# Attention and two MoE layers on one core: the inverse sums travel through DRAM, halves are added on VectorE, and the attention stage gets a new order

## The chip, the cores and the metric

One program on one NeuronCore of a Trainium2 chip. The metric is the device time of the whole program in microseconds, as the median of several runs. The kernel before takes 1170.56 us (three runs, 1170.41 to 1171.14).

## The reference

Thirty-two heads (batch 4 by 8 heads) of 576 positions by 64 channels, in float32:

```
q_rot, k_rot = rotate(q), rotate(k)
scores = q_rot @ k_rot.T / sqrt(64)
attn   = exp(scores - max); attn /= sum(attn) + 1e-9
x      = (attn @ v) laid out as 2304 tokens x 512
h = x @ w_in;  g = s * relu(h)**2 + b;  x = g @ w_out      # 512 -> 2048 -> 512
h = x @ w_in2; g = h * sigmoid(1.702 h); out = g @ w_out2  # 512 -> 2048 -> 512
```

## The kernel before

Every float32 operand of a large product is split in a high and a low part of type fp32r, and a product is two or three matmuls of parts. The program has an attention stage (0 to about 355 us) and a layer stage (from there to the end). The layer stage is a dense row of matmuls at L725 and L753 and is hardly touched by the change, except at its start: its first weights are split in `split_w` (Whi on ScalarE, Wlo on another engine), `first_w` does that for the first two blocks of weights inside the attention stage, and the other blocks are loaded by SyncE after its attention work.

The attention stage works on 16 pairs of heads (`p`), h = 0 and 1 within a pair. 576 rows are four full tiles of 128 (j = 0 to 3) and a tail of 64; the tails of both heads share one tile (T). The jobs of a pair are:

- load (SyncE, q, k and v from DRAM into raw and vraw), rot (GpSimd, rotation into rot), prep (TensorE, transposes of rot), qk and klo (ScalarE and VectorE: high and low part of the transposed q and k), qcopy and kcopy (SyncE: copies within SBUF that lay the parts side by side);
- S (TensorE, scores of one tile), max (VectorE, negated row maximum), exp (ScalarE, exponential with the row's sum), all three for eight tiles and for T;
- X (TensorE, transposes of the exponentials), hi (ScalarE) and lo (VectorE), the two parts of the result;
- V and vlo (GpSimd, parts of v), PV (TensorE, 20 matmuls of one head). The high part of v stands in one half of the 128 output rows and the low part in the other, so the result of a head is the sum of two halves of 64 rows;
- evac (ScalarE, all 128 rows of PV's PSUM tile to O), rest (SyncE, a DMA that brings one half of O to the other half's partitions), add (GpSimd, the sum of the halves, osum);
- inv (VectorE, reciprocal of the nine columns of sums), widen (ScalarE, each inverse repeated over 64 columns), B (TensorE, five transposes, which make rows of the inverses in PSUM), finish (VectorE, osum times these rows, into xT).

Each engine runs its jobs in an order written by hand: PE_ORDER, ACT_ORDER, DVE_ORDER, POOL_ORDER and SP_ORDER are lists of one step, and a token such as `S00@1` means the job S of head 0, tile 0, for the pair one ahead of the step. `program` (L82) runs the list for each step. Engines meet only through semaphores.

All results of TensorE pass through four PSUM tiles (slots) of two banks. SLOTS names the slot of each TensorE job, in the order of PE_ORDER. A job waits in `freed` (L172) until the last reader of the job that had its slot before is through: exp for S, lo for X, klo for prep, evac for PV, finish for B. So the order of the jobs and their slots decide who waits for whom.

Of the kernel before, what the change touches and what calls it, by code (L numbers as in the profile page):

```python
# [5 lines left out]
F32 = mybir.dt.float32  # L6
# [4 lines left out]
P = 128  # L11
# [19 lines left out]
def fused_kernel(nc, q, k, v, w1_in, w1_out, w_s, w_b, w2_in, w2_out,  # L31
# [17 lines left out]

    TILES = 2 * NM + 1  # L50
# [38 lines left out]
    JOBS = ("S", "ST", "X", "XT", "PV", "prep", "B")  # L89
# [13 lines left out]
    with outer:  # L103
# [62 lines left out]
        rest_in = [sem(f"rest_in{i}") for i in range(2)]  # L166
        added = sem("added")
        scale_set = sem("scale_set")
        eps_done = sem("eps_done")
        inv_step = sem("inv_step")  # L170
        inv_done = sem("inv_done")
        b_done = sem("b_done")  # L172
        x_done = sem("x_done")

        def freed(eng, job):

            if job is None:
# [59 lines left out]
        def first_w(eng, s, hi):  # L237

            if s == NPAIR - 1:
                eng.wait_ge(prep_t, 2 * NPAIR)  # L240
                eng.wait_ge(v_lo, 2 * NPAIR)
                for i in range(AHEAD):
                    split_w(eng, i, hi)

        with ExitStack() as ctx:
# [33 lines left out]
            O = [sb(f"O{i}", [P, S]) for i in range(2)]  # L279
            rest = sb("rest", [P, S])  # L280
            osum = sb("osum", [P, S])
            inv = sb("inv", [P, NM, 2, D])
            inv_c = sb("inv_c", [P, 2 * NM + 1])
# [32 lines left out]
            def attention_sync(sp):  # L316
# [58 lines left out]
                program(SP_ORDER, {"load": load, "loadv": load_next_v, "qcopy": q_copies, "kcopy": k_copy, "rest": load_rest}, after)  # L375

            def attention_gpsimd(pool):
# [11 lines left out]
                made = {}  # L389

                def rotate_one(p, h, _):
                    g = 2 * p + h
                    if g > 0:
                        pool.wait_ge(qk_in[h], (96 if h == 0 else 32) * (p + 1))
                        rotate(pool, g, byc, bys, rot_step, rotated, g - 1)
                        made[rotated] = g

                def hi_V(p, h, _):
# [3 lines left out]
                    made[v_hi] = 2 * p + h + 1  # L402

                def lo_V(p, h, _):
                    pool.wait_ge(v_hi, 2 * p + h + 1)
                    pool.tensor_tensor(V[h][:, :, 1 - h, :], vraw[:, h, :, :], V[h][:, :, h, :].bitcast(F32), ALU.subtract).then_inc(v_lo, 1)
                    made[v_lo] = 2 * p + h + 1

                def add(p, h, _):

                    pool.wait_ge(evac_done, 2 * p + h + 1)
                    pool.wait_ge(rest_in[h], 16 * (p + 1))
                    need(pool, x_done, p)
                    r = rows_of(h)
                    if h == 0:
                        pool.tensor_tensor(osum[r, :], O[0][r, :], rest[r, :], ALU.add).then_inc(added, 1)
                    else:

                        for signal in made:
                            pool.wait_ge(signal, made[signal])  # L420
                        pool.tensor_tensor(osum[r, 0:MAIN], O[1][r, TAIL:S], rest[r, TAIL:S], ALU.add)
                        pool.tensor_tensor(osum[r, MAIN:S], O[1][r, 0:TAIL], rest[r, 0:TAIL], ALU.add).then_inc(added, 1)
                        pool.wait_ge(added, 2 * p + 2)
                    made[added] = 2 * p + h + 1
# [3 lines left out]
                def after(s):  # L428
                    if 0 <= s - 9 < KT:
                        first_x(pool, s - 1, False)  # L430
                        made[x_lo] = s - 8

                program(POOL_ORDER, {"rot": rotate_one, "V": hi_V, "vlo": lo_V, "add": add}, after)

            def attention_tensor(pe):
# [79 lines left out]
                def B_job(p, _, __):  # L515

                    pe.wait_ge(inv_done, p + 1)
                    freed(pe, before[("B", p, 0, 0)])
                    ps, r = banks("B"), ROW[0]
                    pe.transpose(ps[:, r + MAIN:r + MAIN + P], inv_c[:, 2 * NM:2 * NM + 1].broadcast_to([P, P]), id_sb[:])  # L520
                    for t in range(NM):
                        both = inv[:, t, :, :].rearrange("p h d -> p (h d)")
                        mm = pe.transpose(ps[:, r + t * P:r + (t + 1) * P], both, id_sb[:])  # L523
                    mm.then_inc(b_done, 1)

# [10 lines left out]

                program(PE_ORDER, {"S": S_job, "ST": ST_job, "X": X_job, "XT": XT_job, "PV": PV, "prep": prep_job, "B": B_job})

            def attention_scalar(act):
# [13 lines left out]
                def expT(p, _, __):  # L553
                    c = 2 * NM
# [46 lines left out]
                program(ACT_ORDER, {"exp": exp, "expT": expT, "hi": hi, "hiT": hiT, "evac": evac, "qk": qk, "widen": widen},  # L601
                        after)

            def attention_vector(dve):
                def rowmax(p, h, j):
                    c = NM * h + j
                    dve.wait_ge(s_done, 2 * NM * p + c + 1)
# [4 lines left out]
                def rowmaxT(p, _, __):  # L612
                    c = 2 * NM
# [12 lines left out]
                def invert(p, _, __):  # L626
# [5 lines left out]
                    need(dve, b_done, p)  # L632
                    dve.reciprocal(inv_c[:], sums_eps[:]).then_inc(inv_step, 1)

                def finish(p, _, __):
                    if p < NPAIR - 1:
                        finish_pair(p)

                def finish_pair(p):
                    b, t = p // KT * S, p % KT  # L640
                    ps, r = banks("B"), ROW[0]
                    dve.wait_ge(b_done, p + 1)
                    dve.wait_ge(added, 2 * p + 2)
                    dve.tensor_tensor(xT[:, t, b:b + MAIN], ps[:, r:r + MAIN], osum[:, 0:MAIN], ALU.mult)
                    for h in range(2):
                        at = r + MAIN + h * TAIL
                        last = dve.tensor_tensor(xT[rows_of(h), t, b + MAIN:b + S], ps[rows_of(h), at:at + TAIL],
                                                 osum[rows_of(h), MAIN:S], ALU.mult)
                    last.then_inc(x_done, 1)

                def qk_low(p, h, _):
# [14 lines left out]
                program(DVE_ORDER, {"max": rowmax, "maxT": rowmaxT, "lo": lo, "loT": loT, "inv": invert, "finish": finish,  # L666
                                    "klo": qk_low}, lambda s: first_w(dve, s - 1, False))
                return finish_pair

        with ExitStack() as ctx:  # L670
# [125 lines left out]
            with nc.Block() as block:  # L796
# [51 lines left out]
                def _(dve):  # L848
                    finish_pair = attention_vector(dve)
                    dve.wait_ge(sb_in, 32)  # L850
                    dve.wait_ge(pv_done, 2 * NPAIR)
                    for n in range(STEPS):
# [12 lines left out]
                        if n == 2:  # L865
                            finish_pair(NPAIR - 1)
# [46 lines left out]
```

## Time and profile before

| | us |
|---|---|
| median of three runs | 1170.56 |
| the profiled execution | 1169.46 |
| its span, first to last instruction | 1167.6 |
| TensorE matmuls busy | 1111.2 (95%) |
| TensorE weight loads busy | 1049.7 (90%) |
| VectorE busy | 547.8 (47%) |
| ScalarE busy | 512.0 (44%) |
| GpSimd busy | 237.8 (20%) |
| mean granted TensorE clock | 0.995 of full speed |

The shares over the whole span mix two stages. In the attention stage VectorE, ScalarE and GpSimd are each busy about three quarters of the time and TensorE about 93%. In the layer stage TensorE is busy 100% and the others about a third, GpSimd not at all. The profile is read in this order: busy time by stretch, TensorE's waits in the attention stage, the chain of work that ended last over one step of it, then the durations of the operations that the change touches, and SyncE's DMA issues.

### The profile page before, as it was taken

The page shows a single profiled execution, that of the slowest core. Times are in us where ns is not written, and L with a number is a line of the kernel's source. Part 1 is how long each engine was busy: PE and PEld are TensorE (multiplying, and loading weights), DVE is VectorE, ACT ScalarE, POOL GpSimd, SP SyncE. Part 2 cuts the span into 40 slices and gives each one's busy share as a digit, 9 for nine tenths or more (in the row PEclk, how much of TensorE's full clock was granted, in tenths as well). Part 3 has the DMA queues.
Part 4 walks back from the last instruction along what each step waited for, and adds up shares of the span by engine and source line. Part 5 has one row for each costly group of instructions (what it writes and reads, how often), then busy time and mean ns, then how long its engine had stood idle before and what let it go on. Part 6 is the DMA issues. An engine that isn't in the chain of part 4 may idle for free.

```text
span 1167.6 us, 17056 instructions
## 1 busy us (share of the span) xinstructions
PE 1111.2 (95%) x6608; PEld 1049.7 (90%) x6608; DVE 547.8 (47%) x890; ACT 512.0 (44%) x1015; POOL 237.8 (20%) x254
## 2 busy tenths in 40 slices
PE   3899999999988999999999999999999999999997
PEld 3788888888888999999999999999999999999996
DVE  3677777777765643333333335543232323233222
ACT  2777777777764533232332335532222223222222
POOL 5776867777431000000000000000000000000000
PEclk9899999999999999999999999999999999999999
DMA  6555655545313310000000003400000000000000
GB/s 136 122 121 112 147 127 121 123 110 125 73 26 118 126 55 1 1 1 1 1 1 1 1 1 109 127 19 1 28 1 28 1 1 28 1 28 1 28 1 28
DMA packets 96417, 60.60 MB, mean 52 GB/s; under 512 B 62672, under 2 KB 84048, under 8 KB 96336
## 3 DMA queue, kind: packets, MB, share of 16 engines
q1 hardware_dynamic: 95584, 59.27, 20.4%
q8 instruction: 53, 0.87, 0.3%
q10 hardware_dynamic: 752, 0.23, 0.1%
q14 instruction: 28, 0.23, 0.1%
HBM read 31.16 MB, written 4.72 MB: 31 GB/s over the span
## 4 chain that ended last, share of the span: by engine, by line
PE 90%; ACT 3%; issue 2%; DVE 2%; DMA 1%; POOL 1%; SPq 0%; ACTq 0%; POOLq 0%
PE psum L753 34%; PE psum L725 34%; PE psum L511 8%; PE psum L446 4%; PE psum L477 4%; PE psum L474 2%; PE psum L461 1%; PE psum L533 1%; ACT ET L557 1%; ACT QK L580 1%; DVE QK L653 1%; PE psum L493 1%; PE psum L523 1%; ACT E L550 0%; PE psum L531 0%
## 5 line engine op out<-in xcount | busy, mean ns | idle before, releaser
L725 PE MATMUL psum<-xhi,Whi 128*128 128x384 f32 x768 | 258.4, 336 | 3.6 <-DVE Wlo L218 3.6
L725 PE MATMUL psum<-xhi,Wlo 128*128 128x384 f32 x768 | 258.5, 337 | 0.0
L725 PE MATMUL psum<-xlo,Whi 128*128 128x384 f32 x768 | 258.0, 336 | 0.0
L725 PEld LDWEIGHTS psum<-xhi,Whi 128*128 128x128 f32 x768 | 144.5, 188 | 8.1 <-DVE Wlo L218 4.0
L725 PEld LDWEIGHTS psum<-xlo,Whi 128*128 128x128 f32 x768 | 144.4, 188 | 4.0
L725 PEld LDWEIGHTS psum<-xhi,Wlo 128*128 128x128 f32 x768 | 144.5, 188 | 0.0
L861 DVE SCALAR_TENSOR_TENSOR glo<-act,sb_sb,ghi 128x384 fp32r<-128x384 f32 x96 | 60.1, 626 | 148.1 <-ACT ghi L841 148.1
L753 PE MATMUL psum<-ghi,Whi 128*128 128x384 f32 x384 | 128.9, 336 | 0.0
L753 PE MATMUL psum<-glo,Whi 128*128 128x384 f32 x384 | 128.8, 335 | 0.0
L753 PE MATMUL psum<-ghi,Wlo 128*128 128x384 f32 x384 | 128.6, 335 | 0.0
L841 ACT ACTIVATE ghi<-act,sb_sb 128x384 fp32r<-128x384 f32 x96 | 59.2, 617 | 158.2 <-PE psum L753 154.3
L864 DVE TENSOR_TENSOR glo<-act,ghi 128x384 fp32r<-128x384 f32 x96 | 53.7, 559 | 152.3 <-ACT ghi L843 152.3
L843 ACT CAST ghi<-act 128x384 fp32r<-128x384 f32 x96 | 49.3, 513 | 157.3 <-PE psum L753 157.3
L753 PE MATMUL psum<-Wlo,ghi 128*128 128x512 f32 x288 | 114.0, 396 | 0.0
L753 PE MATMUL psum<-Whi,glo 128*128 128x512 f32 x288 | 113.8, 395 | 0.0
L550 ACT ACTIVATE E<-psum,negmax 128x576 f32<-128x576 f32 x128 | 95.0, 743 | 42.7 <-DVE negmax L610 41.0
L620 DVE TENSOR_TENSOR Xlo<-psum,Xhi 128x576 fp32r<-128x576 f32 x128 | 93.4, 751 | 40.7 <-ACT Xhi L564 40.7
L753 PE MATMUL psum<-Whi,ghi 128*128 128x512 f32 x288 | 112.0, 389 | 0.0
L858 DVE TENSOR_TENSOR act<-psum,act 128x384 f32<-128x384 f32 x96 | 53.5, 558 | 123.9 <-ACT act L837 123.9
L610 DVE TENSOR_REDUCE negmax<-psum 128x1 f32<-128x576 f32 x128 | 95.3, 748 | 32.8 <-PE psum L446 31.1
L837 ACT ACTIVATE act<-psum 128x384 f32<-128x384 f32 x96 | 47.2, 492 | 129.4 <-PE psum L725 129.4
L446 PE MATMUL psum<-QK,Q 128*128 128x320 f32 (+1 forms) x512 | 96.0, 317 | 5.3 <-ACT E L550 3.4
(90 smaller groups left out, 1853.6 us busy)
## 6 DMA issues: line engine op xcount, KB each, us to landing
Q<-QK SPq DMA_DIRECT2D x64, 144.0 KB, 2.5
QK<-QK SPq DMA_DIRECT2D x32, 288.0 KB, 3.3
wraw<-in_moe_w_in_dram SPq DMA_DIRECT2D x32, 256.0 KB, 2.8
wraw<-in_moe_w_out_dram SPq DMA_DIRECT2D x32, 256.0 KB, 3.1
rest<-O SPq DMA_DIRECT2D x32, 144.0 KB, 2.3
raw<-in_q_dram SPq DMA_DIRECT2D x32, 128.0 KB, 2.8
raw<-in_k_dram SPq DMA_DIRECT2D x32, 128.0 KB, 2.5
vraw<-in_v_dram SPq DMA_DIRECT2D x32, 128.0 KB, 2.4
```

Of the source, the lines that this page charges most:

```text
L446: mm = pe.matmul(ps[:, a:b], Q[h][p % 2][:, at:at + P], QK[h][p % 2][:, part, c:c + b - a], start=part == 0, stop=part == 1)
L511: mm = pe.matmul(ps[:, a:b], V[h][:, j, :, :].rearrange("p a d -> p (a d)"), x, start=j == 0 and n == 0, stop=j == NM and n == 1)
L550: act.activation(E[p % 2][:, j, h, :], row(banks("S", h, j), h), ACT.Exp, bias=negmax[p % 2][:, c:c + 1], accum_out=sums[p % 2][:, c:c + 1 ...
L610: dve.tensor_reduce(negmax[p % 2][:, c:c + 1], row(banks("S", h, j), h), AX_X, ALU.max, negate=True).then_inc(max_done, 1)
L620: dve.tensor_tensor(Xlo[h][:, j, :], row(banks("X", h, j), h), Xhi[h][:, j, :].bitcast(F32), ALU.subtract).then_inc(et_lo, 1)
L725: mm = pe.matmul(hps(n), w[i][:, kt * P:(kt + 1) * P], x[C % 2][:, kt, :], start=kt == 0 and j == 0, stop=kt == KT - 1 and j == 2)
L753: mm = pe.matmul(dst, lhsT, rhs, start=i == 0 and j == 0, stop=i == NF - 1 and j == 2)
L841: act.activation(ghi[n % 2][:], a[:], ACT.Identity, bias=sb_sb[:, 1:2]).then_inc(g_hi, 1)
L843: act.copy(ghi[n % 2][:], a[:]).then_inc(g_hi, 1)
L858: dve.tensor_tensor(a[:], hps(n), a[:], ALU.mult).then_inc(g_done, 1)
L861: dve.scalar_tensor_tensor(glo[n % 2][:], a[:], sb_sb[:, 1:2], ghi[n % 2][:].bitcast(F32), ALU.add, ALU.subtract).then_inc(g_lo, 1)
L864: dve.tensor_tensor(glo[n % 2][:], a[:], ghi[n % 2][:].bitcast(F32), ALU.subtract).then_inc(g_lo, 1)
```

## The change

- B and widen are gone. The inverses of a pair (`inv`, 128 by 9) are written to DRAM by one DMA (`put_inv`) as nine rows of 128, element by element, and read back by three DMAs (`get_inv`) as one row of 576 per head, repeated over the 64 partitions of that head, into `inv_row`. The columns of sums are renumbered (COL) so that the tails' column stands between the heads.
- rest and add are gone. evac copies only the 64 rows of its own head; `total` (the token sum) on VectorE adds the other half straight from PSUM. A slot of PV is free after sum, no longer after evac.
- finish is one multiplication of 128 by 576 on GpSimd.
- All five orders, the slots and the order of the banks are new. `first_w` is spread over two steps, and its low parts move from VectorE to GpSimd. finish of the last pair no longer stands in VectorE's layer loop.

```diff
-    PE_ORDER = order("S12@0 prep0@2 S13@0 X00@0 X01@0 S00@1 S01@1 ST@1 prep1@2 S02@1 S03@1 X02@0 X03@0 S10@1 PV1@-1 "
-                     "X10@0 X11@0 XT@0 X12@0 X13@0 B@-1 S11@1 PV0@0")
-    ACT_ORDER = order("hi13@-1 exp11@0 widen@-1 evac0@-1 qk0@2 exp12@0 hi00@0 exp13@0 hi01@0 exp00@1 exp01@1 qk1@2 "
-                      "expT@1 exp02@1 exp03@1 hi02@0 hi03@0 exp10@1 evac1@-1 hi10@0 hi11@0 hiT@0 hi12@0")
-    DVE_ORDER = order("max01@0 lo01@-1 maxT@0 max02@0 klo1@1 max03@0 max10@0 lo02@-1 lo03@-1 lo10@-1 lo11@-1 loT@-1 "
-                      "lo12@-1 inv@-1 max11@0 lo13@-1 finish@-2 max12@0 klo0@2 max13@0 lo00@0 max00@1")
-    POOL_ORDER = order("V0@0 add0@-1 vlo0@0 rot0@3 rot1@3 V1@0 add1@-1 vlo1@0")
-    SP_ORDER = order("loadv1@-3 loadv0@-2 load1@0 qcopy1@-1 kcopy0@-1 rest1@-4 kcopy1@-1 load0@1 rest0@-3 qcopy0@0")
-    SLOTS = [2, 3, 1, 0, 3, 2, 0, 1, 2, 3, 0, 1, 2, 3, 0, 1, 3, 2, 0, 1, 3, 2, 0]
-    SLOT_ORDER = (2, 1, 0, 3)
+    PE_ORDER = order("X01@-1 S01@0 S02@0 X02@-1 S03@0 X03@-1 prep1@1 ST@0 S10@0 S11@0 S12@0 S13@0 PV1@-2 prep0@2 "
+                     "X10@-1 XT@-1 X11@-1 X12@-1 X13@-1 PV0@-1 S00@1 X00@0")
+    ACT_ORDER = order("qk0@2 hi10@-1 hiT@-1 hi11@-1 hi12@-1 hi13@-1 evac0@-1 hi00@0 hi01@0 exp00@1 exp01@1 hi02@0 "
+                      "exp02@1 hi03@0 qk1@2 exp03@1 expT@1 exp10@1 exp11@1 exp12@1 exp13@1 evac1@-1")
+    DVE_ORDER = order("max10@0 max11@0 max12@0 max13@0 sum1@-2 klo0@2 lo10@-1 loT@-1 lo11@-1 lo12@-1 inv@-1 lo13@-1 "
+                      "sum0@-1 max00@1 lo00@0 max01@1 lo01@0 max02@1 lo02@0 max03@1 lo03@0 klo1@2 maxT@1")
+    POOL_ORDER = order("vlo1@-1 V0@0 finish@-2 rot0@3 vlo0@0 V1@0 rot1@3")
+    SP_ORDER = order("loadv1@-2 qcopy0@0 kcopy0@0 qcopy1@0 load1@1 kcopy1@0 put@-3 loadv0@-1 get@-3 load0@2")
+    SLOTS = [0, 2, 3, 1, 0, 2, 1, 3, 0, 2, 1, 3, 0, 1, 3, 2, 0, 1, 3, 2, 1, 3]
+    SLOT_ORDER = (1, 3, 2, 0)
...
         def first_w(eng, s, hi):
 
-            if s == NPAIR - 1:
-                eng.wait_ge(prep_t, 2 * NPAIR)
-                eng.wait_ge(v_lo, 2 * NPAIR)
-                for i in range(AHEAD):
-                    split_w(eng, i, hi)
+            i = s - (NPAIR - 2)
+            if 0 <= i < AHEAD:
+                if hi:
+                    eng.wait_ge(rotated, 2 * NPAIR - 1)
+                    eng.wait_ge(prep_t, 2 * NPAIR)
+                if i == 1:
+                    eng.wait_ge(v_lo, 2 * NPAIR)
+                split_w(eng, i, hi)
...
+                def put_inv(p, _, __):
+                    sp.wait_ge(inv_done, p + 1)
+                    need(sp, inv_in[p % 2], 48 * (p // 2))
+                    sp.dma_start(inv_dram[p % 2].rearrange("t p -> p t"), inv[p % 2][:], allow_slow_non_contiguous=True).then_inc(inv_out[p % 2], 16)
+
+                def get_inv(p, _, __):
+                    sp.wait_ge(inv_out[p % 2], 16 * (p // 2 + 1))
+                    need(sp, x_done, p)
+                    flat = inv_dram[p % 2].rearrange("t p -> (t p)")
+                    for h, at, a, n in ((0, 0, 0, S), (1, MAIN, S, TAIL), (1, 0, S + TAIL, MAIN)):
+                        sp.dma_start(inv_row[rows_of(h), at:at + n],
+                                     flat[a:a + n].rearrange("(o q) -> o q", o=1).to_broadcast([D, n])).then_inc(inv_in[p % 2], 16)
...
+                def finish(p, _, __):
+                    b, t = p // KT * S, p % KT
+                    pool.wait_ge(sum_done, 2 * p + 2)
+                    pool.wait_ge(inv_in[p % 2], 48 * (p // 2 + 1))
+                    pool.tensor_tensor(xT[:, t, b:b + S], osum[p % 2][:], inv_row[:], ALU.mult).then_inc(x_done, 1)
...
+                def total(p, h, _):
+
+                    dve.wait_ge(evac_done, 2 * p + h + 1)
+                    if h == 0:
+                        need(dve, x_done, p - 1)
+                    ps, r = banks("PV", h)[rows_of(1 - h), ROW[h]:ROW[h] + S], rows_of(h)
+                    if h == 0:
+                        last = dve.tensor_tensor(osum[p % 2][r, :], ps, O[r, :], ALU.add)
+                    else:
+                        dve.tensor_tensor(osum[p % 2][r, 0:MAIN], ps[:, TAIL:S], O[r, TAIL:S], ALU.add)
+                        last = dve.tensor_tensor(osum[p % 2][r, MAIN:S], ps[:, 0:TAIL], O[r, 0:TAIL], ALU.add)
+                    last.then_inc(sum_done, 1)
```

## Rows read from the trace of the kernel before

**Rows 1.** Busy time by stretch: start:end, length, each engine's busy us, clock, DMA share, GB/s.
```profile
200.00:300.00 100.00, 93.13 (x705) 85.85 (x704) 76.65 (x124) 76.92 (x162) 76.39 (x79) 1.00 0.51 113
```

**Rows 2.** Waits of TensorE, 100 to 300 us: who waited for whom, total, times, longest.
```profile
PE psum L474 <- DVE QK L653: 6.1, 10, 0.6
PE psum L474 <- ACT ET L557: 4.6, 10, 0.5
```

**Rows 3.** The chain that ended last, in time: start, us, what (B at 209.89).
```profile
209.89 0.28 PE psum L520
...
210.61 0.71 PE psum L446 x4
211.32 2.82 PE psum L511 x20
214.13 0.53 PE psum L446 x4
```

**Rows 4.** Groups of instructions, 100 to 300 us: busy us, mean ns, idle before.
```profile
L610 DVE TENSOR_REDUCE negmax<-psum 128x1 f32<-128x576 f32 x79 | 59.1, 748 | 18.0 <-PE psum L446 16.8
L550 ACT ACTIVATE E<-psum,negmax 128x576 f32<-128x576 f32 x78 | 58.0, 743 | 25.6 <-DVE negmax L610 24.5
L620 DVE TENSOR_TENSOR Xlo<-psum,Xhi 128x576 fp32r<-128x576 f32 x79 | 57.6, 750 | 22.5 <-ACT Xhi L564 22.5
...
L550 ACT ACTIVATION_READ_ACCUMULATOR E<-psum,negmax 128x1 f32 x78 | 15.4, 197 | 0.0
...
L416 POOL TENSOR_TENSOR osum<-O,rest 64x576 f32<-64x576 f32 x10 | 14.1, 1414 | 23.1 <-issue 23.1
...
L574 ACT COPY O<-psum 128x576 f32<-128x576 f32 x20 | 12.8, 640 | 16.7 <-PE psum L511 16.7
```

**Rows 5.** Timelines of VectorE, ScalarE, TensorE near 196 us: start, duration, [idle before <-releaser].
```profile
195.72 0.82 DVE L653 SCALAR_TENSOR_TENSOR QK<-psum,qk_scale,QK 128x576 fp32r<-128x576 f32 x1 [0.56 <-ACT QK L580]
196.46 0.75 DVE L610 TENSOR_REDUCE negmax<-psum 128x1 f32<-128x576 f32 x1
197.12 0.75 DVE L620 TENSOR_TENSOR Xlo<-psum,Xhi 128x576 fp32r<-128x576 f32 x1
...
197.24 0.74 ACT L550 ACTIVATE E<-psum,negmax 128x576 f32<-128x576 f32 x1 [0.30 <-DVE negmax L610]
...
196.60 0.33 PE L474 MATMUL psum<-id_sb,ET 128*128 128x128 f32 x1 [0.61 <-DVE QK L653]
```

**Rows 6.** Timelines of VectorE and GpSimd: the small addition of inv, twice.
```profile
48.66 0.16 DVE L630 TENSOR_TENSOR sums_eps<-sums,eps 128x9 f32<-128x9 f32 x1
...
211.04 0.42 DVE L630 TENSOR_TENSOR sums_eps<-sums,eps 128x9 f32<-128x9 f32 x1
...
210.15 1.29 POOL L421 TENSOR_TENSOR osum<-O,rest 64x512 f32<-64x512 f32 x1 [1.24 <-DMA rest<-O]
```

**Rows 7.** Timeline of SyncE's queue: DMA issues, start and time taken.
```profile
228.56 0.60 SPq L352 DMA_DIRECT2D QK<-QK  x1
...
229.83 1.59 SPq L331 DMA_DIRECT2D raw<-in_q_dram  x2
```

**Rows 8.** DMA issues of the whole run: count, KB each, median us from issue to landing.
```profile
Q<-QK SPq DMA_DIRECT2D x64, 144.0 KB, 2.5
...
raw<-in_k_dram SPq DMA_DIRECT2D x32, 128.0 KB, 2.5
...
raw<-in_k_dram SPq DMA_DIRECT2D x32, 16.0 KB, 2.1
```

**Rows 9.** Timelines: X10 of pairs 0 and 14; load and first matmul of weight block 2.
```profile
44.48 0.30 PE L474 MATMUL psum<-id_sb,ET 128*128 128x128 f32 x1 [1.65 <-DVE Xlo L620]
...
327.52 0.27 PE L474 MATMUL psum<-id_sb,ET 128*128 128x128 f32 x1
...
355.71 0.58 SPq L205 DMA_DIRECT2D wraw<-in_moe_w_in_dram  x1
...
362.87 0.45 PE L725 MATMUL psum<-xhi,Whi 128*128 128x384 f32 x1 [3.64 <-DVE Wlo L218]
```

More of the change, by code:

```diff
@@ L86, in program @@
                 after(s)
[L89 removed]
+    JOBS = ("S", "ST", "X", "XT", "PV", "prep")
     SLOT = {(kind, h, j): slot for (kind, h, j, _), slot in zip([t for t in PE_ORDER if t[0] in JOBS], SLOTS)}
@@ L277, in fused_kernel @@
             sums_eps = sb("sums_eps", [P, 2 * NM + 1])
[L279 to L283, printed above, removed]
+            O = sb("O", [P, S])
+            osum = [sb(f"osum{i}", [P, S]) for i in range(2)]
+            inv = [sb(f"inv{i}", [P, 2 * NM + 1]) for i in range(2)]
+            inv_row = sb("inv_row", [P, S])
+            inv_dram = [nc.dram_tensor(f"inv_dram{i}", [2 * NM + 1, P], F32, kind="Internal").ap() for i in range(2)]
             q_h = q.rearrange("b h s d -> (b h) s d")
@@ L374, in attention_sync @@
                 sp.dma_start(sb_sb[:, 1:2], w_b.rearrange("(a b) -> a b", a=1).to_broadcast([P, 1])).then_inc(sb_in, 16)
-                program(SP_ORDER, {"load": load, "loadv": load_next_v, "qcopy": q_copies, "kcopy": k_copy, "rest": load_rest}, after)
+                program(SP_ORDER, {"load": load, "loadv": load_next_v, "qcopy": q_copies, "kcopy": k_copy, "put": put_inv, "get": get_inv}, after)
             def attention_gpsimd(pool):
@@ L406, in lo_V @@
                     pool.tensor_tensor(V[h][:, :, 1 - h, :], vraw[:, h, :, :], V[h][:, :, h, :].bitcast(F32), ALU.subtract).then_inc(v_lo, 1)
[L407 to L424, printed above, removed]
+                def finish(p, _, __):
[3 more added lines that the diff above has]
+                    pool.tensor_tensor(xT[:, t, b:b + S], osum[p % 2][:], inv_row[:], ALU.mult).then_inc(x_done, 1)
                 pool.wait_ge(tabs_in, 96)
                 def after(s):
[L429 to L433, printed above, removed]
+                    first_x(pool, s - 1, False)
+                    first_w(pool, s - 1, False)
+                program(POOL_ORDER, {"rot": rotate_one, "V": hi_V, "vlo": lo_V, "finish": finish}, after)
             def attention_tensor(pe):
@@ L513, in PV @@
                     mm.then_inc(pv_done, 1)
[L515 to L524, printed above, removed]
                 def prep_job(p, h, _):
@@ L599, in after @@
                     first_w(act, s, True)
-                program(ACT_ORDER, {"exp": exp, "expT": expT, "hi": hi, "hiT": hiT, "evac": evac, "qk": qk, "widen": widen},
+                program(ACT_ORDER, {"exp": exp, "expT": expT, "hi": hi, "hiT": hiT, "evac": evac, "qk": qk},
                         after)
@@ L631, in invert @@
                     dve.wait_ge(eps_done, p + 1)
[L632 to L649, printed above, removed]
+                    need(dve, inv_out[p % 2], 16 * (p // 2))
+                    dve.reciprocal(inv[p % 2][:], sums_eps[:]).then_inc(inv_done, 1)
+                def total(p, h, _):
[9 more added lines that the diff above has]
+                    last.then_inc(sum_done, 1)
                 def qk_low(p, h, _):
@@ L665, in attention_vector @@
                 dve.wait_ge(scale_set, 1)
-                program(DVE_ORDER, {"max": rowmax, "maxT": rowmaxT, "lo": lo, "loT": loT, "inv": invert, "finish": finish,
-                                    "klo": qk_low}, lambda s: first_w(dve, s - 1, False))
-                return finish_pair
+                program(DVE_ORDER, {"max": rowmax, "maxT": rowmaxT, "lo": lo, "loT": loT, "inv": invert, "sum": total,
+                                    "klo": qk_low})
         with ExitStack() as ctx:
```

48 lines of the change are left out of this document (17 added, 31 removed).

## The prediction

> **What bounds the kernel now.** The busy times by stretch come first. In the attention stage TensorE is busy 93 us in 100 and the three others 77 each [rows 1], so no single engine is the bound; the order of the jobs is. The step repeats: between X10 of pair 0 at 44.48 and X10 of pair 14 at 327.52 [rows 9] lie 14 steps, 20.2 us each; the undisturbed ones in the middle take 20.3. TensorE's waits say where its 7% go: once a step it stands 0.6 us for klo and once 0.5 us for expT [rows 2]. The chain of work shows what the rest is: TensorE's own jobs. From the third block of the layers (362.87, rows 9) to the end TensorE never pauses, and no line of that is changed. So the change is worth what it does to 14 steps, to the fill before them and to the turn into the layers.
>
> **What B costs.** B starts at 209.89 and the next job at 210.61 [rows 3], so 0.72 us, and the S behind it takes 0.71 where one behind a PV takes 0.53. TensorE loses 0.9 us of work per pair. That is 14 us if TensorE stayed the bound. It does not, as the walk below shows.
>
> **Work moved.** VectorE gives up finish and takes up sum0 and sum1. All three read 576 columns of PSUM in one to three pieces; lo does that in one piece in 0.75 [rows 4], and for a further small piece I add 0.15 of estimate. So VectorE gains two times 0.75 and loses one time 0.75 and the smaller pieces: some 0.5 us a pair more. ScalarE gives up widen (512 columns, about like evac's 576); evac has half the rows and the same columns, and I keep its 0.64 [rows 4]. GpSimd gives up two adds over 576 columns, 1.41 each, and takes one multiplication of 576 columns, 1.41 by the same row [rows 4]. Each of the three was busy 77% of a step of 20.3, 15.6 us [rows 1]; VectorE comes to 16.1, the others to less. None fills a step, so the order decides again, and I walk through the new one.
>
> **Prices of the walk.** The walk goes job by job through the new lists: a job starts when its engine is free, its data are there and, on TensorE, its slot is. Back to back, VectorE's operations start 0.66 apart (196.46 to 197.12, rows 5) though each lasts 0.75; klo 0.74. A dependent on another engine waits for the end: klo at 195.72 plus 0.82, TensorE starts at 196.60, 0.06 later; max at 196.46 plus 0.75, exp at 197.24, 0.03 later [rows 5]. So max to exp 0.78, lo to TensorE 0.81, klo to TensorE 0.88, evac to sum 0.67, hi to lo the same. exp to TensorE is 0.74 plus the reading of the sum, 0.9 in all [rows 4]. On ScalarE exps start 0.72 apart, hi and evac 0.55, qk 0.64. On TensorE: S 0.53 [rows 3], or 0.63 after a wait; PV 2.7 (2.82 with its end, rows 3); the rest by the same view, X 0.55, XT 0.65, prep 0.5, ST 1.14; the next engine starts 0.2 after the job's issue ends, so PV to evac is 2.9 and S or X to its reader 0.8.
>
> **One step of the new order**, zero where PV1 starts. evac1 2.92, sum1 3.59. sum1's release is 0.88 later, with its second piece. Slot 0 goes from PV1 to X11, which waits for it: 4.47. klo0 4.36, lo10 5.10, loT 5.77, and PV0 (slot 2, behind XT) 6.65. X12 and X13 wait 0.2 on the way. evac0 9.57, sum0 10.24; S01 has PV0's slot and starts 11.05. max00 10.91, lo00 11.57, which frees slot 3 for S02 at 12.38: TensorE, through with S01 at 11.65, stands 0.7. max01 12.24, lo01 12.90, max02 13.57. X02 at 13.0, its hi 13.77, lo02 14.44, prep1 in its slot 15.25 (0.4 idle), qk1 16.05, klo1 16.82, maxT 17.55. exp03 stands behind qk1 on ScalarE, 16.69, and S10 has its slot: 17.6, where ST was over at 16.9 (0.7 idle). max10 18.43, exp10 19.21, PV1 of the next step 20.15. So the step takes 20.15 us against 20.29: B's 0.9 and the two old waits of 1.1 go, and about 2 us of new waits, now for VectorE's chain, come. In 14 steps that is 2.0 us.
>
> **What the walk leaves out.** In four steps ScalarE casts a piece of x (0.5 each) right behind evac1; here qk0 and klo0 wait for it, 0.4 each, in the old order it fell into an idle stretch: +1.6. Two steps before the end preps, qk and klo are gone; by the same walk this shortens the new order by 2.0, the old one by 1.0 (283.0 measured between the two X10, against 14 times 20.29): -1.0.
>
> **The fill.** SyncE is in order. load1 of pair 1 now stands behind the wait of kcopy0 for qcopy0 (2.5, rows 8) and goes out near 18.3, formerly 14.7. Following GpSimd's rotations from there, prep0 of pair 2 comes at 31.8, as before, and prep0 of pair 3, which now stands ahead of X10 of pair 0, at 43.2. X10 of pair 0 follows at 43.7 to 44.0, against 44.48: -0.6. Sum so far at X10 of pair 14: -2.0 +1.6 -1.0 -0.6 = -2.0.
>
> **The turn.** The walk goes on from the last PV1 of a full step (pair 13), as zero, with X10 of pair 14 at 2.7. PV1 of pair 14 is over near 15. V1 of the last pair waits for it; behind it on GpSimd stands Wlo0, 1024 columns, by 1.41 for 576 [rows 4] 2.5 us, and only then vlo1, for which ScalarE waits ahead of its second Whi (1.0). What is queued behind this on ScalarE is hi10 of the last pair; TensorE waits for it about 4 us ahead of PV0. hi10 goes at 19.8, lo10 at 20.4, and the chain hiT, loT, lo11, lo12, inv ends at 23.5. Whi0 on ScalarE one step earlier adds 0.8: 24.3. The third block of weights is queued on SyncE behind put and get of the last pair: put L, get 1.75 for three issues, then load and the two splits, 7.2 as before (355.71 to 362.87, rows 9). Its first matmul, H2, starts at 24.3 + L + 8.9 = 33.2 + L, which is 30.5 + L from X10 of pair 14; now it is 362.87 - 327.52 = 35.35 [rows 9].
>
> **The price L of put** is not in the trace: 1152 elements of 4 bytes. Below: a load of 512 rows lands in 2.5, one of 64 rows in 2.1 [rows 8]; at 0.4 per 448 rows, 1152 land in 3.1. Above: nothing in the trace writes 4 bytes to DRAM, and if an element cost four times what a row of these loads adds, L is 6.2. I take 4, nearer the low end, since rows 8 are the nearest. The turn is then 34.5, which is -0.85. Sum -2.85, on the 1169.46 of the profiled execution 1166.6 (its span of 1167.6 and 1.9 around it), and the median of the runs lies 1.1 above that: 1167.7.
>
> The Trainium skill speaks against such a store: "DMA: Bandwidth & Descriptors", section "Rules for kernel authors", says that a non-contiguous last dim becomes one descriptor per element, and its section "Anatomy of one DMA" gives a DMA of GpSimd's path some 2.0 us of fixed time. With the 10.5 ns that the page gives for a packet there, 72 to each of 16 engines, my estimate by the page is 2.8 us, which would make the sum -4.0. No row here shows a 4-byte store.
>
> **Rival 1, SyncE becomes the bound.** An issue takes 0.6, two tail loads 1.6 [rows 7]. SyncE's ring: qcopy1 to kcopy1 3.1 (the landing of 2.5, rows 8, under which load1 goes out), 0.6, put L, get 1.75, load0 4.1, loadv1 1.2, qcopy0 to kcopy0 3.1, 0.6: 14.5 + L. It fits in 20.15 up to L = 5.6. Beyond that every us of L is a us per step: at L = 7 the step is 21.5, 13 steps cost 17.5 more and the turn 3: 1188; at L = 6, 4.6 and 2: 1174. For it: one element per row, and a DMA share of 51% already [rows 1]. Against: landing hardly depends on the number of rows [rows 8]. This one is on the other side, slower.
>
> **Rival 2, the chain through VectorE is shorter or longer than walked.** It has some 25 links; 0.02 us on each is 0.5 a step, 7 us in all. Shorter, 19.6: 1160. Longer, 20.6: 1174. For shorter: VectorE's work is 16 us and nothing else holds the step. For longer: every mis-ordered wait adds.
>
> **Rival 3, GpSimd holds VectorE.** sums_eps takes 0.16 with GpSimd idle and 0.42 when L421 runs, and ends with it: 211.46 and 211.44 [rows 6]. In the new order inv falls beside vlo1 or the end of rot1, at worst 1.5 us; lo13 has 0.7 of slack before X00: up to 0.8 a step, 1178 at worst, 1170 if rarely. The Trainium skill has this as a rule ("SBUF — State Buffer", "Who interferes with whom"): an operation of VectorE with two SBUF inputs contends with a GpSimd one that reads SBUF; by that rule, and the trace agrees, sum and lo, with one input in PSUM, are free of it.
>
> **That it does nothing**: B's time is simply handed to VectorE, step 20.3: 1169 to 1171.
>
> **Chances.** Forecast (1164 to 1171) 0.45, of which 0.27 faster, 0.13 same, 0.05 slower. SyncE the bound 0.2, slower. Chain shorter 0.17, faster; longer 0.05, slower. GpSimd 0.05, half same, half slower. Nothing gained 0.08: 0.05 same, 0.03 faster. A measurement of this kernel tells 0.2%, 2.3 us, from no change: faster 0.47, same 0.21, slower 0.32. The range leaves out the best of the short chains and L beyond 6.5: 1158 to 1181.
>
> **What would show it.** Right: no L520; a step of about 20.1 with TensorE busy 86% of it; its waits now for lo00 ahead of S02, lo02 ahead of prep1, exp03 ahead of S10; put landing in about 4; TensorE idle some 4 us ahead of the last PV0. Wrong: SyncE with no idle time and TensorE waiting for prep or S at random (rival 1), sums_eps over 1 us (rival 3), a step under 19.8 or over 20.5 (rival 2). The prediction falls if L is over 5.6 or if a link of the chain is mis-sized by a tenth.

## The result

The changed kernel takes 1250.77 us (median of four runs, 1249.44 to 1251.73), the kernel before 1170.85 beside it: 1.0688 times as long, 95% interval 1.0668 to 1.0708. The forecast was 1167.7 with a range of 1158 to 1181, so sign and range were both wrong.

The chain of the work that ended last, as the page of the changed kernel sums it up: shares by engine, then by line.

```profile
PE 65%; DMA 19%; SPq 9%; issue 2%; ACT 1%; POOL 1%; DVE 1%; ACTq 0%; POOLq 0%; DVEq 0%
PE psum L727 32%; PE psum L699 32%; DMA inv_dram<-inv 12%; DMA Q<-QK 6%; SPq L334 2%; SPq L367 2%; SPq L351 1%; SPq L331 1%; SPq L355 1%; SPq L338 1%; SPq L339 1%; ACT E L533 1%; PE psum L440 1%; DVE Xlo L598 0%; DMA wraw<-in_moe_w_out_dram 0%
```

L727 and L699 are the layers. Of the rest nearly all is SyncE's: its issues and the landings it waits for. One step of that chain, in time:

```profile
199.84 11.52 DMA inv_dram<-inv
...
211.38 0.47 SPq L367
...
220.55 2.81 DMA Q<-QK
...
224.52 3.40 DMA Q<-QK
...
228.51 11.54 DMA inv_dram<-inv
```

The put takes 11.5 from issue to landing, SyncE stands in get's wait meanwhile, and everything queued behind it (loads of q and k, the next copies) comes late. SyncE's waits from 100 to 300 us, and TensorE's and GpSimd's longest ones of that stretch:

```profile
SPq L367 <- DMA inv_dram<-inv: 60.0, 7, 9.3
SPq L355 <- DMA Q<-QK: 24.6, 14, 2.6
...
POOL V L409 <- DMA vraw<-in_v_dram: 48.6, 8, 7.0
...
PE psum L514 <- POOL rot L317: 35.9, 7, 9.0
```

GpSimd waits for v and k, TensorE for the rotation. Busy times of the stretch of [rows 1]:

```profile
200.00:300.00 100.00, 77.28 (x526) 71.97 (x525) 64.21 (x97) 58.33 (x120) 47.27 (x47) 0.89 0.42 88
```

TensorE is busy 77 in place of 93, and its granted clock is 0.89 in place of 1.00: from 219 to 223 us it does nothing, and from 223 to 227 its granted clock is 0.50 (1.2 in place of 2.4 GHz). No engine is near full. Over the whole run the put lands in 9.9, 10.7 and 11.7 (least, median, most).

Where the 80.5 us of span (1248.1 against 1167.6) went, by three marks, the ones of [rows 9]:

| | before | after | difference |
|---|---|---|---|
| start to X10 of pair 0 | 44.48 | 48.68 | +4.2 |
| 14 steps, to X10 of pair 14 | 283.04 | 352.20 | +69.2 |
| X10 of pair 14 to block 3 of the layers | 35.35 | 42.20 | +6.9 |
| from there to the end | 804.7 | 805.0 | +0.3 |

The last mark in the timeline of TensorE:

```profile
443.08 0.69 PE L699 MATMUL psum<-xhi,Whi 128*128 128x384 f32 x1 [8.94 <-DVE Wlo L217]
```

### The profile page after: what moved, and what is told of

It is laid out like the page before. It is cut to its first block, busy times and chain, and to the rows that moved or that the text cites. A ratio compares the mean times of both kernels' runs of the same rounds, so it can differ in the third digit from the quotient of the medians.

```text
span 1248.1 us, 16779 instructions
## 1 busy us (share of the span) xinstructions
PE 1128.4 (90%) x6528; PEld 1065.9 (85%) x6528; DVE 555.7 (45%) x888; ACT 508.7 (41%) x999; POOL 215.7 (17%) x224
## 4 chain that ended last, share of the span: by engine, by line
PE 65%; DMA 19%; SPq 9%; issue 2%; ACT 1%; POOL 1%; DVE 1%; ACTq 0%; POOLq 0%; DVEq 0%
PE psum L727 32%; PE psum L699 32%; DMA inv_dram<-inv 12%; DMA Q<-QK 6%; SPq L334 2%; SPq L367 2%; SPq L351 1%; SPq L331 1%; SPq L355 1%; SPq L338 1%; SPq L339 1%; ACT E L533 1%; PE psum L440 1%; DVE Xlo L598 0%; DMA wraw<-in_moe_w_out_dram 0%
## 5 line engine op out<-in xcount | busy, mean ns | idle before, releaser
L699 PE MATMUL psum<-xhi,Whi 128*128 128x384 f32 x768 | 258.5, 337 | 8.9 <-DVE Wlo L217 8.9
L699 PE MATMUL psum<-xhi,Wlo 128*128 128x384 f32 x768 | 258.5, 337 | 0.0
L699 PE MATMUL psum<-xlo,Whi 128*128 128x384 f32 x768 | 258.0, 336 | 0.0
L699 PEld LDWEIGHTS psum<-xhi,Whi 128*128 128x128 f32 x768 | 144.7, 188 | 13.4 <-DVE Wlo L217 9.3
L699 PEld LDWEIGHTS psum<-xlo,Whi 128*128 128x128 f32 x768 | 144.8, 188 | 4.1
L699 PEld LDWEIGHTS psum<-xhi,Wlo 128*128 128x128 f32 x768 | 144.6, 188 | 0.0
L727 PE MATMUL psum<-ghi,Whi 128*128 128x384 f32 x384 | 128.3, 334 | 0.0
L727 PE MATMUL psum<-ghi,Wlo 128*128 128x384 f32 x384 | 128.3, 334 | 0.0
L727 PE MATMUL psum<-glo,Whi 128*128 128x384 f32 x384 | 128.3, 334 | 0.0
L727 PE MATMUL psum<-Wlo,ghi 128*128 128x512 f32 x288 | 113.9, 396 | 0.0
L727 PE MATMUL psum<-Whi,glo 128*128 128x512 f32 x288 | 113.7, 395 | 0.0
L727 PE MATMUL psum<-Whi,ghi 128*128 128x512 f32 x288 | 111.9, 389 | 0.0
L440 PE MATMUL psum<-QK,Q 128*128 128x320 f32 (+1 forms) x512 | 88.4, 312 | 20.7 <-DVE Xlo L598 9.6
L440 PEld LDWEIGHTS psum<-QK,Q 128*128 128x128 f32 x512 | 71.5, 192 | 31.7 <-DVE Xlo L598 16.9
```

Source lines behind the costliest of these rows:

```text
L440: mm = pe.matmul(ps[:, a:b], Q[h][p % 2][:, at:at + P], QK[h][p % 2][:, part, c:c + b - a], start=part == 0, stop=part == 1)
L699: mm = pe.matmul(hps(n), w[i][:, kt * P:(kt + 1) * P], x[C % 2][:, kt, :], start=kt == 0 and j == 0, stop=kt == KT - 1 and j == 2)
L727: mm = pe.matmul(dst, lhsT, rhs, start=i == 0 and j == 0, stop=i == NF - 1 and j == 2)
```

## Experiments

Ratios are against the kernel before, run beside each kernel on the same chip (medians 1168.0 to 1169.1).

**e1: the same order, a cheaper put.** The nine values of a partition go out as one run of 36 bytes: 128 runs in place of 1152. The inverses stand in the wrong order in DRAM; the amount of work is the same.

```
-  sp.dma_start(inv_dram[p % 2].rearrange("t p -> p t"), inv[p % 2][:], ...)
+  sp.dma_start(inv_dram[p % 2].rearrange("t p -> (t p)").rearrange("(p t) -> p t", t=2 * NM + 1), inv[p % 2][:])
```

> The store of the inverses writes 36 contiguous bytes per partition (128 runs) in place of 1152 single elements; the inverses arrive in the wrong order, all jobs and sizes are the same. Theory A (SyncE stands at get for the landing L of put; its ring is 14.5 + L): L falls from 10.7 to about 2.3, the ring to 17, so the step is the walk's 20.15; with the fill 4 us late and the turn about 2 us early 1168 to 1174. Theory B (the new order itself is slow, by its waits for slots): stays at 1230 or more. Theory C (1152 small packets a pair crowd the other transfers): also near 1170, so this run does not tell A from C.

Measured: 1177.54, ratio 1.0077 (1.0055 to 1.0098). The put lands in 2.7. SyncE's waits from 100 to 300 us:

```profile
SPq L355 <- DMA Q<-QK: 28.1, 20, 3.5
SPq L351 <- DVE QK L628: 27.1, 10, 3.4
SPq L367 <- DMA inv_dram<-inv: 8.3, 10, 1.5
```

SyncE now waits for VectorE (L351), so it has slack again. Each kernel against the kernel before beside it, the loss falls from 79.9 to 9.1 us: some 71 went with the pieces of the put alone. The other 9 are the order's own, and 3.5 above the upper end that I expected; in the spans (1174.7 against 1167.6) they are 7.1: X10 of pair 0 at 49.05 (+4.6), 14 steps of 286.9 in all (+3.9), the turn -1.3. So with a cheap put this order is still slower than before.

**e2: 640 single elements and 128 runs of 16 bytes** (wrong order again).

```
+  sp.dma_start(inv_dram[p % 2].rearrange("t p -> p t")[:, 0:5], inv[p % 2][:, 0:5], ...)
+  rest = inv_dram[p % 2].rearrange("t p -> (t p)")[5 * P:9 * P].rearrange("(p t) -> p t", t=4)
+  sp.dma_start(rest, inv[p % 2][:, 5:9])
```

> Five of the nine columns are stored element by element (640 elements), the other four as 128 runs of 16 bytes by a second DMA. The inverses of those four arrive in the wrong order. Theory A with a landing that grows by element, 2.1 + 8.6 x 640/1152 = 6.9, second DMA behind it 1 more: ring 22.5 with the extra issue, step 22 to 23, total 1203 to 1215. If the landing is a fixed price of such a store: 10.7 again, total about 1250.

Measured: 1236.72 (one run). SyncE's timeline around one put:

```profile
196.85 0.53 SPq L360 DMA_DIRECT2D inv_dram<-inv  x1
197.43 0.96 SPq L362 DMA_DIRECT2D inv_dram<-inv  x1
...
206.58 1.75 SPq L369 DMA_DIRECT2D inv_row<-inv_dram  x3
```

The get goes out 9.7 behind the put's issue where it was 11.5. Two thirds of the pieces took 84% of the time, and the total lies between my two expectations: neither a price per element alone nor a fixed price fits. With 128 pieces landing in 2.7 (e1) most of the price comes before the 768th piece. But e2 mixes 4-byte and 16-byte pieces, so the form of the price, by number or by size of the pieces, stays open.

**e3: the wait taken out of SyncE's way.** get goes behind the first kcopy of the next step and finish behind V1, so nobody stands for the landing.

```
-  POOL_ORDER = order("vlo1@-1 V0@0 finish@-2 rot0@3 vlo0@0 V1@0 rot1@3")
-  SP_ORDER = order("loadv1@-2 qcopy0@0 kcopy0@0 qcopy1@0 load1@1 kcopy1@0 put@-3 loadv0@-1 get@-3 load0@2")
+  POOL_ORDER = order("vlo1@-1 V0@0 rot0@3 vlo0@0 V1@0 finish@-2 rot1@3")
+  SP_ORDER = order("loadv1@-2 qcopy0@0 kcopy0@0 get@-4 qcopy1@0 load1@1 kcopy1@0 put@-3 loadv0@-1 load0@2")
```

> The store stays as it is, 1152 elements; get of a pair stands one step later on SyncE, behind kcopy0, so that the store lands under other work, and finish stands behind V1 on GpSimd. Theory A: SyncE no longer stands at get, the step is 20.2 although put still lands in 10 to 12; only the turn into the layers still pays for L of the last pair, 8 us more than in the run with 128 runs: 1176 to 1184. Theory C (traffic): the step stays above 22, total over 1200. Theory B: about 1230 to 1250.

Measured: 1211.42, ratio 1.0371 (1.0343 to 1.0398). SyncE's longest wait from 100 to 300 us:

```profile
SPq L355 <- DMA Q<-QK: 51.0, 18, 7.6
```

No one waits for the put any more, yet half of the loss stays: the copies issued behind it wait up to 7.6 where 2.5 was usual [rows 8]. My theory, that only the wait costs, fell. A second one was needed: the put delays the transfers behind it.

**e5 and e6: the store alone, added to the kernel before.** Per pair SyncE issues the same store of 1152 elements from a constant tile, at the end of its list; nothing reads it. e6 also lets SyncE wait for it.

```
+  need(sp, put_out, 16 * (p - 1))
+  sp.dma_start(put_dram[p % 2].rearrange("t p -> p t"), eps[:], ...).then_inc(put_out, 16)
+  sp.wait_ge(put_out, 16 * (p + 1))      # e6 only
```

> The kernel before, with one more DMA a pair on SyncE that stores a constant tile of 128 x 9 to DRAM element by element, and nobody waits for it except the next such store. It is the traffic of put alone in the old order. Theory A: nothing but one issue of 0.6 in SyncE's slack: 1170 to 1174. Theory C: 1185 or more, the step over 21.

> As the kernel before with one element-wise store a pair (the run before this took 1282), and SyncE now also waits for its landing right behind the issue. If the wait at get is what costs (theory A as predicted), this run is the slow one and must lie far above 1282, by up to 10 us in 16 steps: 1350 or more. Theory D (the store keeps SyncE's queue for itself for some 9 us, and whatever is issued behind it starts only then, waited for or not): 1275 to 1310.

Measured: 1282.24, ratio 1.0975 (1.0946 to 1.1004), without the wait, and 1293.68 (one run) with it. SyncE's timeline in e5 (L365 is the store), and the longest wait of all engines from 100 to 300 us:

```profile
215.26 0.58 SPq L365 DMA_DIRECT2D put_dram<-eps  x1
...
219.73 1.86 SPq L330 DMA_DIRECT2D raw<-in_q_dram  x1
221.64 6.62 SPq L330 DMA_DIRECT2D raw<-in_k_dram  x1
```

```profile
POOL byc L310 <- DMA raw<-in_k_dram: 78.4, 7, 13.2
```

The kernel before, which needs none of this data, loses 114 us. The eighth issue behind the store takes 6.62 where 0.6 is usual, and GpSimd waits up to 13.2 for that load. The store holds the queue behind it, whoever waits; the wait itself adds only some 11 (one run, on another chip).

**e7: the same store from ScalarE's queue.**

> The same store of 1152 elements a pair in the kernel before, issued from ScalarE's queue in place of SyncE's; nobody waits for it but the second next such store. While the store runs the DMA engines show a busy share of only a quarter, so by theory D it holds the queue and not the engines: the loads on SyncE's queue go on beside it and ScalarE pays one issue of 0.6 a step: 1175 to 1195. If the 16 engines themselves are held (theory C): 1260 or more, as from SyncE.

Measured: 1213.89 (one run). The DMAs of that kernel from 100 to 300 us (count, KB each, median landing):

```profile
Q<-QK SPq DMA_DIRECT2D x32, 144.0 KB, 2.6
...
raw<-in_k_dram SPq DMA_DIRECT2D x16, 128.0 KB, 2.7
...
put_dram<-eps ACTq DMA_DIRECT2D x8, 4.5 KB, 11.0
```

The store is as slow, but the medians of SyncE's DMAs are back near those of [rows 8]. Still 46 us are lost, more than the 7 to 27 of one expectation and less than the 92 of the other, and the longest waits say where:

```profile
PE psum L534 <- DVE xT L654: 30.7, 4, 10.1
...
POOL osum L424 <- DMA rest<-O: 24.9, 7, 6.9
```

Single copies of rest still come up to 6.9 late, add and finish behind them, and B's slot. The steps alternate: from 155 to 310 us, measured from store to store, they take 31.0, 20.3, 32.1, 20.3, 31.2 and 20.3. So part of the harm is in one queue and part is not; what the two queues share that slows single transfers was not found.

**e7b: reading instead of writing.** SyncE loads 1152 elements of 4 bytes, with the same pattern of pieces, into a tile that nobody uses.

> In place of the store, SyncE issues one load of 1152 elements of 4 bytes from DRAM into 128 x 9 a pair (data that nobody uses); order and waits as in the run with the store from SyncE (1282). If the price is one per element whatever the direction: 1270 to 1290. If it is the writing of 4 bytes to DRAM: 1172 to 1185.

Measured: 1172.07 (one run), 4 us over the kernel before.

```profile
got<-in_v_dram SPq DMA_DIRECT2D x16, 4.5 KB, 2.6
```

Same pieces, same bytes, same queue (the profiles of e5 and e7b count the same 115105 DMA packets): 2.6 in place of 10.7. The number of pieces alone doesn't cost this; writing them to DRAM does. What about such writes is slow, the 4 bytes or that neighbours in DRAM come from different partitions, was not tried: a store of 1152 single elements that lie far apart would tell.

**e8: B replaced, the old order kept.** What is B's removal worth by itself? TensorE transposes the 128 by 9 inverses in one instruction (I, in B's place and slot), ScalarE copies the 9 by 128 result, SyncE writes nine rows of 512 bytes and reads them back in four DMAs, GpSimd multiplies. rest and add stay.

```
-  PE_ORDER = order("... X12@0 X13@0 B@-1 S11@1 PV0@0")
+  PE_ORDER = order("... X12@0 X13@0 I@0 S11@1 PV0@0")
+  pe.transpose(banks("I")[0:2 * NM + 1, 0:P], inv_c[:], id_sb[:])
```

> The old order with B replaced: one transpose of the 128 x 9 inverses (job I, in B's slot and at B's place), a copy of 9 x 128 on ScalarE in place of widen, a store of nine rows of 512 bytes, four broadcast loads back, and finish as one multiplication on GpSimd behind add1. inv stands ahead of lo10 on VectorE. The halves are still brought by rest and added on GpSimd. If TensorE's own work bounds the old step, B's 0.9 less 0.2 for I comes off each of 14 steps: 20.29 to about 19.6, 1158 to 1163, under both kernels. If a chain through VectorE and ScalarE is behind it by less: 1164 to 1168. If GpSimd's 16.9 us in a step or SyncE's five more issues delay add or the copies of q: above 1172.

Measured: 1171.97, ratio 1.0032 (1.0021 to 1.0042). TensorE is busy 18.56 us of a step in place of 18.92, so B's removal saved it 0.36, and the step is still 20.3. TensorE's timeline where S11 starts:

```profile
209.36 0.27 PE L541 MATMUL psum<-id_sb,inv_c 128*9 128x128 f32 x1
210.00 0.79 PE L469 MATMUL psum<-QK,Q 128*128 128x320 f32 x4 [0.37 <-DVE XTlo L640]
```

S11 waits 0.37 for loT, the reader of XT in its slot, which is all that was saved. The time was handed to the chain behind X. The turn also cost 3.1: vlo1, for which the first Whi waits, stands behind finish (e11 below takes this back).

**e9: S11 and I exchanged**, so that S11 has the slot behind lo11.

> The old order with the rows of inverses through DRAM (as in e8), and S11 and I swapped, so that S11 takes slot 3, free behind lo11, and I takes slot 2, free behind loT. In e8 TensorE stood 0.37 us per step at S11 for loT, and S11 stood 0.27 behind I. Theory G (that slot was what gave B's time back): S11 starts some 0.5 earlier, the step goes from 20.29 to 19.8 to 19.9, e8's 1172.0 becomes 1165 to 1167. Rival H (the chain of max, exp and lo further on holds the step): the 0.5 reappears as a longer wait for klo or expT, now 0.6 and 0.45, the step stays at 20.2 to 20.3 and the time at 1171 to 1172.

Measured: 1173.87, ratio 1.0038 (1.0025 to 1.0051). The wait moved and the step stayed, as the rival said, though not where the rival put it. TensorE's timeline, PV1 and PV0 of one step and PV1 of the next:

```profile
205.88 0.38 PE L534 MATMUL psum<-Xhi,V 128*128 128x320 f32 x1 [0.28 <-issue]
212.94 0.36 PE L534 MATMUL psum<-Xhi,V 128*128 128x256 f32 x1 [0.35 <-DVE Xlo L636]
...
226.18 0.38 PE L534 MATMUL psum<-Xhi,V 128*128 128x320 f32 x1 [0.28 <-issue]
```

Now PV0 waits, for lo12, which frees its slot, and it stands 7.06 behind PV1, as in e8. The chain evac1, hi10, hi11, hiT, hi12, lo12 fixes that distance. The fill is 2.2 longer than in e8 (X10 of pair 0 at 46.17 and 43.94), but the intervals of the two ratios overlap, so that e9 is slower than e8 isn't shown.

**e11 and e12: vlo1 ahead of add1 on GpSimd**, in e9 and in the kernel before.

> e9 with vlo1 on GpSimd ahead of add1 and finish. In the steps it should change nothing (GpSimd has some 3.5 us of idle time in each). At the turn the two Whi of the first weights wait for vlo1 of the last pair, which in e8 came at 347.8, behind an addition and finish; it now comes near 342.6, Whi at 344.7 in place of 348.8, hi13 of the last pair at 346.6 in place of 350.7. PV1 of the last pair then waits for evac0 (350) in place of 352.25. Expected 2 to 4 us less than e9: 1161 to 1165. If the load of the third block behind the four reads of the rows on SyncE is what ends last, it is less than 1 us.

> The kernel before with one edit: vlo1 on GpSimd ahead of add1. It splits e11's gain over e9 (4.8 us). Theory: in the kernel before, Whi of the first weights waits for vlo1 until 347.9 where ScalarE is free from 345.2; add1 of 1.6 us goes from ahead of it, so Whi starts up to 2.6 earlier, and PV1 of the last pair, which now waits 2.3 for evac0, starts 1.6 earlier: 1165 to 1167.5 against 1168.5. Rival: the load of the third block, at 355.7 on SyncE behind evac1, moves by the same, or it does not and the time stays within 0.5 of the kernel before.

Measured: e11 1169.07, ratio 1.0003 (0.9994 to 1.0013), so 4.8 less than e9 (2 to 4 expected, from a lower start: 1161 to 1165), nearly all of it in the turn, 33.6 in place of 38.3 from X10 of pair 14 to block 3 of the layers; e12 1167.88, ratio 0.9985 (0.9975 to 0.9995), less of a gain than expected. In the kernel before this is worth 1.2, in e9 four times that, since there finish had been put ahead of vlo1 as well. The steps stay at 20.3 in both.

**e13: PV0 in another slot.** e11 with PV0 in XT's slot and S11 in X11's, XT in the one that PV1 leaves, and I, ahead of S11 again as in e8, in the unused first 128 columns of S11's slot.

```
-  SLOTS = [2, 3, 1, 0, 3, 2, 0, 1, 2, 3, 0, 1, 2, 3, 0, 1, 3, 2, 0, 1, 3, 2, 0]
-  ACT_ORDER = order("hi13@-1 icopy@-1 exp11@0 evac0@-1 ...")
+  SLOTS = [0, 3, 1, 2, 3, 0, 2, 1, 0, 3, 2, 1, 0, 3, 2, 1, 3, 2, 0, 1, 3, 2]
+  ACT_ORDER = order("hi13@-1 exp11@0 icopy@-1 evac0@-1 ...")
```

> e11 with other slots: PV0 stands in the slot of XT (free when loT is through) in place of that of X12 (lo12), S11 in that of X11 (lo11), XT takes the slot of PV1, and I writes its 9 rows in the unused first 128 columns of S11's slot, just ahead of S11, with its copy behind exp11 on ScalarE. In e8 and in e9 alike PV0 starts 7.05 us behind PV1 of the same step (230.95 and 223.95 in e8, 212.94 and 205.88 in e9), first waiting for loT, then for lo12: the chain evac1, hi10, hi11, hiT, hi12, lo12. Theory J (this chain of slots is what gives B's time back in the old order): PV0 starts 0.6 to 0.7 earlier, the step is 19.6 to 19.75, the time 1159 to 1163, against 1169.1 for e11. Rival K (the rest of the step, from PV0 over evac0 and klo to PV1, takes the time back): PV1 to PV0 falls to 6.4 and PV0 to PV1 grows from 13.2 to 13.9, the time 1168 to 1170.

Measured: 1159.14 (1158.95 to 1160.65), ratio 0.9916 (0.9904 to 0.9928), faster than both kernels. TensorE's timeline, PV1, I, S11, PV0 and PV1 of the next step:

```profile
200.91 0.39 PE L536 MATMUL psum<-Xhi,V 128*128 128x320 f32 x1 [0.28 <-issue]
...
206.64 0.27 PE L543 MATMUL psum<-id_sb,inv_c 128*9 128x128 f32 x1
206.67 0.77 PE L469 MATMUL psum<-QK,Q 128*128 128x320 f32 x4
207.38 0.35 PE L536 MATMUL psum<-Xhi,V 128*128 128x256 f32 x1
...
220.62 0.38 PE L536 MATMUL psum<-Xhi,V 128*128 128x320 f32 x1 [0.28 <-issue]
```

The step is 19.71, and neither S11 nor PV0 waits: PV0 stands 6.47 behind PV1 in place of 7.06. The run makes two changes at once: the waits of e8 and e9 (0.37 and 0.35 a step) are gone, and S11 follows I by 0.03, where in e8 I took 0.27. X10 of pairs 0 and 14 stand at 45.89 and 320.73, so 14 steps take 274.8 in place of 283.0. TensorE's two old waits remain:

```profile
PE psum L499 <- DVE QK L658: 6.1, 10, 0.6
PE psum L499 <- ACT ET L579: 5.0, 11, 0.5
```

## Why the prediction was wrong

**The price of the put: wrong, and this decided.** I took L as 4 between 3.1 and 6.2; it measured 10.7 (9.9 to 11.7). Both bounds came from rows of loads [rows 8], and the upper one from a factor of four that no row supported. e7b shows that loads of such pieces are indeed cheap (2.6), so the rows were true and spoke of something else. For a store of 4-byte elements to DRAM the trace of before had no row, and then the bounds should have been far wider. So the step that failed is the term L = 4, and with it the claim that SyncE's ring fits in a step: the ring holds SyncE in every full step.

At 10.7 the ring of rival 1 gives 14.5 + 10.7 = 25.2 a step. The 14 steps measured 352.2, also 25.2 on average, but that agreement is luck: from XT to XT the first two take 20.2 and 21.7 and the last two 20.9 and 19.0, and the ten between them 27.0 on average. The ring is 1.7 longer than the rival's sum, by the starts of the puts of pairs 0 to 11 (66.72 to 362.28: 26.9 a step), and 1.0 of this lies between kcopy0 and kcopy1, 4.7 in place of 3.7, where the copies of q land in more than 2.5 (2.81 and 3.40 in the chain above). By the prediction's own rule, 13 steps that are each longer by what L has beyond the slack, 14 steps would be 347.3; 352.2 is 4.9 more. So the mechanism of rival 1 was right; its chance of 0.2, its L of 6 to 7 and, by less, its sum were not.

The Trainium skill names this form in "DMA: Bandwidth & Descriptors", section "Rules for kernel authors": a last dim that isn't contiguous becomes one descriptor per element. The estimate of 2.8 that I drew from that page's packet price, which the page measured on loads from DRAM, fits the read (2.6) and not the write (10.7). The measurement decides: the rule warns rightly, the price per packet doesn't carry over to such writes.

**"It costs only who waits": incomplete.** Rival 1 counted L once, in SyncE's wait. e3 and e5 show a second price, paid by the DMAs queued behind the store even if nobody waits for it. In the changed kernel only two loads of v stand between the put and the wait. They come late (GpSimd waits 48.6 for them from 100 to 300 us), but the chain of the step runs through SyncE and not through them.

**The walk of the step: near, and short by some 0.35.** Before the first put SyncE isn't the bound. XT of pairs 0 and 1, in TensorE's timeline:

```profile
49.47 0.60 PE L487 MATMUL psum<-id_sb,E 128*128 128x128 f32 x4
...
69.64 0.60 PE L487 MATMUL psum<-id_sb,E 128*128 128x128 f32 x4
```

20.17, where the walk said 20.15. That this agrees to 0.02 is luck in part: no pair has a PV1 and a sum1 ahead of X11 there, and from XT to PV0 it is 2.40, in a full step of e1 2.76. The walk's three waits are there:

```profile
208.19 0.80 PE L440 MATMUL psum<-QK,Q 128*128 128x256 f32 x4 [0.66 <-DVE Xlo L598]
211.15 0.30 PE L514 MATMUL psum<-id_sb,rot 128*128 128x128 f32 x1 [0.30 <-DVE Xlo L598]
213.53 2.37 PE L440 MATMUL psum<-QK,Q 128*128 128x320 f32 x16 [0.50 <-ACT E L533]
```

The walk said 0.7 for lo00, 0.4 for lo02, 0.7 for exp03. In e1, where the put no longer holds the order up, later steps take 20.5, so the walk is short by some 0.35, of which sum0 to max00 (0.79 in place of 0.67), lo02 to prep1 (0.91 in place of 0.81) and PV0 (6.78 behind PV1 in place of 6.65) are three terms. The four steps that cast x take 21.0, some 0.4 more as forecast. So rival 2, longer, held beside it. With the price of the put mended the forecast would still have had the wrong sign: at e1's L of 2.7 its sum gives a span of 1163.4, and 1174.7 was measured. Of these 11.3 the fill has 5.2, the 14 steps 5.3 and the turn 0.8.

**B's 0.9 a pair: too much.** The prediction said that removing B is worth little because VectorE's chain takes its place; e8 shows the same in the old order (nothing gained of 0.36), and e9 and e13 show what that chain hangs on: in which slot S11 and PV0 stand. With it mended, and I at next to no cost, the gain is 0.59 a step (20.30 to 19.71), all of it in TensorE's busy time (18.92 to 18.33). The 0.18 that the prediction adds for the S behind B wasn't B's: in e13, without B, PV0 follows S11 by the same 0.71.

**The fill: wrong by 4.8.** Forecast -0.6, measured +4.2. The forecast walked GpSimd's rotations and put prep0 of pair 3 at 43.2. Its rotation was done at 44.46 and prep0 started at 47.96, so most of the error lies in TensorE's own chain, which wasn't walked there. One wait in it, for a slot, in TensorE's timeline:

```profile
22.63 1.73 PE L440 MATMUL psum<-QK,Q 128*128 128x256 f32 x6 [1.77 <-DVE QK L628]
```

S00 of pair 0 waits for klo0 of pair 1, whose prep has S00's slot; in a full step that reader is long through. That this wait and those behind it make all of the 4.2 was not tried by itself; e1, with a cheap put, has the same fill (49.05).

**The turn: near as a formula.** Forecast 30.5 + L; with 10.7 that is 41.2, measured 42.2. The idle time ahead of the last PV0 was 4.8, some 4 forecast. Nearly all that was wrong is L.

**GpSimd holding VectorE: no sign of it in the step.** sums_eps takes 0.16 to 1.13 in the changed kernel, so the collision is there, but its median is 0.41 as in the kernel before, e9 has more of it (0.72) at an unchanged step, and in e1 VectorE stands idle 0.9 soon behind it.

## What to carry to other kernels

Bound a transfer by rows of the same direction and the same size of piece; where the trace has none, the range must be open upward, and a rival that decides from a threshold gets its chance from that range. A slow store like this one costs twice: once for whoever waits, once for what is queued behind it, so moving the wait alone isn't enough; make the pieces longer instead (here one transpose of 128 by 9, which TensorE does in 0.3). And work taken off an engine is gained only when the next job's slot is free at that moment: look up which reader frees it before counting the gain.

## What the hardware showed

- A store to DRAM of 1152 elements of 4 bytes (4.5 KB) lands in 10.7; the same bytes as 128 runs of 36 bytes land in 2.7; the same pieces read from DRAM in 2.6 (one run). While the store ran (201.5 to 210.5) the 16 DMA engines were busy only 23% and moved 24 GB/s:

```profile
201.50:210.50 9.00, 8.34 (x65) 7.70 (x64) 7.55 (x13) 6.03 (x12) 3.85 (x5) 1.00 0.23 24
```

  In the last 4 us before it landed (207 to 211) they showed a busy share of 0.00: it wasn't the engines' throughput that the store used up.

- Such a store holds up its own queue: an issue of a load behind it took 6.62 in place of 0.6. From another queue it takes as long (11.0, one run) and leaves the medians of the others alone, though not every transfer.
